# Attention and two MLPs on one core: SP's loads reordered, additions moved, x divided in place, and the query's low half later in VectorE's round

## The reference

```python
scores = scale * q @ k.T                    # causal
cum = cumsum(max(s, 0)); bias = min(-(cum[i] - cum[j]), 0)
attn = softmax(where(causal, -1e9, scores + bias))      # sum + 1e-9
x = (attn @ v) put back as (2304 tokens, 512)
h = x @ w_in; solu = h * softmax(h)                     # w_in 512 x 1024
x2 = ((solu - mean) / sqrt(var + 1e-6) * g_ln) @ w_out  # w_out 1024 x 512
y = max(x2 @ w1, x2 @ w2, x2 @ w3) @ w_out2             # w1..w3 512 x 768
```

## Time and profile before

| | us |
|---|---|
| three runs | 772.12, 773.01, 778.30 |
| median | 773.01 |
| profiled execution | 773.02 |
| its span (first to last instruction) | 771.2 |
| TensorE busy | 722.3 (94%) |
| VectorE, ScalarE, POOL busy | 394.9, 327.0, 251.4 |

### The profile page before, as it was taken

The page is one execution under the profiler, slowest core; times in us unless marked ns, Lnnn a source line. Parts: engine busy times, 40 slices in busy tenths (PEclk is TensorE's granted clock), DMA queues, the critical chain, the costliest instruction groups (busy, mean ns, idle before and its releaser), DMA issues.

```text
span 771.2 us, 12703 instructions
## 1 busy us (share of the span) xinstructions
PE 722.3 (94%) x4248; PEld 664.4 (86%) x4248; DVE 394.9 (51%) x702; ACT 327.0 (42%) x795; POOL 251.4 (33%) x248
## 2 busy tenths in 40 slices
PE   2799999999878899999999999999999999999997
PEld 2788888888767688989898989999989999899995
DVE  8898988888853675636354364612203213132120
ACT  1798888898853443424233242412112112121111
POOL 6766779888872842606040200000000000000000
PEclk9999999999998999999999999999999999999999
DMA  6598887878765312306100031000010000100101
GB/s 142 114 215 195 198 184 181 186 185 190 160 146 113 84 35 48 82 1 170 36 0 0 0 106 59 1 14 28 1 42 1 13 29 1 38 2 0 41 0 41
DMA packets 58227, 59.42 MB, mean 77 GB/s; under 512 B 23572, under 2 KB 45204, under 8 KB 58164
## 3 DMA queue, kind: packets, MB, share of 16 engines
q1 hardware_dynamic: 58196, 59.02, 32.0%
HBM read 44.15 MB, written 10.10 MB: 70 GB/s over the span
## 4 chain that ended last, share of the span: by engine, by line
PE 71%; DVE 8%; issue 6%; POOL 5%; DMA 4%; ACT 3%; SPq 2%; DVEq 0%; POOLq 0%; ACTq 0%
PE ps L652 10%; PE ps L653 10%; PE ps L651 10%; PE ps L584 4%; PE ps L586 4%; PE ps L585 4%; DMA qk_raw<-in_qk_dram 4%; PE ps L572 3%; PE ps L574 3%; PE ps L573 3%; PE ps L664 3%; PE ps L665 3%; PE ps L666 3%; PE ps L481 3%; DVE lnT_lo L1170 1%
## 5 line engine op out<-in xcount | busy, mean ns | idle before, releaser
L653 PE MATMUL ps<-x_lo,w_hi 128*128 (+1 forms) x432 | 144.4, 334 | 0.0
L651 PE MATMUL ps<-x_hi,w_hi 128*128 128x384 f32 x432 | 144.4, 334 | 0.0
L652 PE MATMUL ps<-x_hi,w_lo 128*128 128x384 f32 x432 | 144.4, 334 | 0.0
L481 PE MATMUL ps<-ident,probs 128*128 128x128 f32 x480 | 78.2, 289 | 21.9 <-DVE pt_lo L1069 15.6
L844 ACT ACTIVATE probs<-ps,nmax 128x576 f32<-128x576 f32 (+4 forms) x160 | 83.0, 539 | 17.7 <-DVE nmax L1062 17.5
L1069 DVE TENSOR_TENSOR pt_lo<-ps,pt_hi 128x512 fp32r<-128x512 f32 (+1 forms) x128 | 78.3, 652 | 11.6 <-ACT pt_hi L854 8.3
L481 PEld LDWEIGHTS ps<-ident,probs 128*128 128x128 f32 x480 | 52.4, 144 | 33.9 <-DVE pt_lo L1069 21.7
L651 PEld LDWEIGHTS ps<-x_hi,w_hi 128*128 128x128 f32 x432 | 81.1, 188 | 0.2
L652 PEld LDWEIGHTS ps<-x_hi,w_lo 128*128 128x128 f32 x432 | 81.1, 188 | 0.2
L653 PEld LDWEIGHTS ps<-x_lo,w_hi 128*128 128x128 f32 x432 | 81.1, 188 | 0.0
L854 ACT ACTIVATE pt_hi<-ps 128x512 fp32r<-128x512 f32 (+1 forms) x128 | 69.9, 572 | 26.4 <-PE ps L481 22.6
(11 more groups left out here) (101 smaller groups left out, 1436.3 us busy)
## 6 DMA issues: line engine op xcount, KB each, us to landing
qk_raw<-in_qk_dram SPq DMA_DIRECT2D x64, 288.0 KB, 4.4
xT<-halves SPq DMA_DIRECT2D x32, 144.0 KB, 2.5
xb_dram<-halves SPq DMA_DIRECT2D x32, 144.0 KB, 2.4
xb<-xb_dram SPq DMA_DIRECT2D x24, 192.0 KB, 3.9
rinvB<-rsum_dram SPq DMA_DIRECT2D x24, 192.0 KB, 4.1
stage<-in_moe_w_dram SPq DMA_DIRECT2D x18, 256.0 KB, 4.3
out_dram<-stage SPq DMA_DIRECT2D x18, 256.0 KB, 2.0
v_raw<-in_v_dram SPq DMA_DIRECT2D x32, 128.0 KB, 4.1
```

The source lines that it names most:

```text
L481: mm = pe.transpose(ps[:, GBANK[g], P * n:P * (n + 1)], probs[1 - par][:, o:o + P], ident[:, :])
L651: pe.matmul(dst, w_hi[f][:, i, c, :], x2_hi[par][:, c, :], start=(c == 0), stop=False)
L652: pe.matmul(dst, w_lo[f][:, i, c, :], x2_hi[par][:, c, :], start=False, stop=False)
L653: mm = pe.matmul(dst, w_hi[f][:, i, c, :], x2_lo[:, c, bass.ds(g * GT, GT)], start=False, stop=(c == KC - 1))
```

## The change

SP: aux(t-1) is loaded behind qk(t) and v(t-2), so SP no longer waits in `reload(t)` for the scores of head t-2. The list of the last heads is in another order. There are two `rinvB`, and `xg` is gone: `divide` writes back into `xT`, and no longer waits for `x_low`. POOL does round 30 before `join(0)`, and `divide(0)` before round 31. VectorE's `q_low(t+1)` stands behind `pt_low` 0 and 1.

```diff
@@ SP
+            def reload_aux(t, par):
+                sp.wait_ge(scores_done, 3 * (t - 1))
+                load_aux(t, par)
+
             def reload(t, par, known=None):
...
                 load_qk(t, par)
                 if known is None or known >= 4:
                     reload_v(t - 2, par)
-                if known == 2:
+                if known == 3:
                     sp.wait_ge(aux_stored, 16)
-                sp.wait_ge(scores_done, 3 * (t - 1))
-                load_aux(t, par)
+                if known is None or known >= 3:
+                    reload_aux(t - 1, 1 - par)
                 if known is None or known >= 5:
                     store_x(t - 5, 1 - par)
...
             reload(HEADS - 4, 0)
             load_xb(0)
             reload(HEADS - 3, 1)
             reload(HEADS - 2, 0)
+            reload(HEADS - 1, 1)
             sp.wait_ge(rinv_done, 1)
             store_rinv(slice(0, LAST))
-            reload(HEADS - 1, 1)
+            reload_aux(HEADS - 1, 1)
+            reload_v(HEADS - 2, 0)
+            store_x(HEADS - 5, 1)
             sp.wait_ge(rinv_stored, 16 * NCH)
             load_rinv(0)
-            load_xb(1)
-            reload_v(HEADS - 2, 0)
-            store_x(HEADS - 5, 1)
             reload_v(HEADS - 1, 1)
             store_x(HEADS - 4, 0)
+            load_rinv(1)
+            load_xb(1)
             store_x(HEADS - 3, 1)
+            store_x(HEADS - 2, 0)
             load_xb(2)
             sp.wait_ge(xg_ready, 1)
-            load_rinv(1)
-            store_x(HEADS - 2, 0)
+            load_rinv(2)
             store_x(HEADS - 1, 1)
             sp.wait_ge(rinv_done, 2)
             store_rinv(slice(LAST, HEADS))
             sp.wait_ge(rinv_stored, 16 * 2 * NCH)
-            for g in range(2, NG):
-                sp.wait_ge(xg_ready, g)
+            for g in range(3, NG):
+                load_xb(g)
+                sp.wait_ge(xg_ready, g - 1)
                 load_rinv(g)
-                if g + 1 < NG:
-                    load_xb(g + 1)
@@ POOL
-            def divide(g, known):
+            def divide(g, par):
                 cols = xT[:, :, bass.ds(g * GT, GT)]
-                pool.wait_ge(rinvB_loaded, 64 * (g + 1))
-                if known != 0:
-                    pool.wait_ge(x_lo_ready, 3 * g)
+                pool.wait_ge(rinvB_loaded[par], (g - par) * 32 + 64)
                 pool.wait_ge(x_added, g + 1)
-                pool.tensor_tensor(xg[:, :, :], cols, rinvB[:, :, :], ALU.mult).then_inc(xg_ready, 1)
+                pool.tensor_tensor(cols, cols, rinvB[par][:, :, :], ALU.mult).then_inc(xg_ready, 1)
...
+            slot(HEADS - 2, 0, HEADS - 2)
             join(0)
-            slot(HEADS - 2, 0, HEADS - 2)
+            divide(0, 0)
             slot(HEADS - 1, 1, HEADS - 1)
             join(1)
-            divide(0, 0)
             slot(HEADS, 0, HEADS)
-            divide(1, None)
+            divide(1, 1)
             join(2)
@@ VectorE
             def slot(t, par, known):
-                if live(known, -1):
-                    q_low(t + 1, 1 - par)
                 if live(known, 0):
                     row_max(t, par, 4)
                     row_max(t, par, 0)
                     row_max(t, par, 3)
                 if live(known, 1):
                     pt_low(0, t, par, known)
                     pt_low(1, t, par, known)
+                if live(known, -1):
+                    q_low(t + 1, 1 - par)
```

More of the change, by code:

```diff
@@ L111, in attention_and_mlp @@
         ab_.__enter__()
-        rinvB = sb(ab_, "rinvB", [P, KC, GT])
-        xg = sb(ab_, "xg", [P, KC, GT])
+        rinvB = [sb(ab_, f"rinvB{i}", [P, KC, GT]) for i in range(2)]
         xb = sb(ab_, "xb", [P, KC, GT])
@@ L220, in attention_and_mlp @@
         wout_lo_ready = sem("wout_lo_ready")
-        rinvB_loaded = sem("rinvB_loaded")
+        rinvB_loaded = [sem(f"rinvB_loaded{i}") for i in range(2)]
         xg_ready = sem("xg_ready")
@@ L393, in load_rinv @@
                         src = rsum_dram[HB * b_:HB * (b_ + 1), s0:s0 + GT // 2].rearrange("(j r) t -> r j t", r=2)[par:par + 1]
-                        dst = rinvB[D * par:D * (par + 1), :, part * GT // 2:(part + 1) * GT // 2]
-                        sp.dma_start(dst, src.broadcast_to([D, KC, GT // 2])).then_inc(rinvB_loaded, 16)
+                        dst = rinvB[g % 2][D * par:D * (par + 1), :, part * GT // 2:(part + 1) * GT // 2]
+                        sp.dma_start(dst, src.broadcast_to([D, KC, GT // 2])).then_inc(rinvB_loaded[g % 2], 16)
             LAST = HEADS - HB
@@ L811, in group @@
                 if more and not first:
-                    divide(g + 1, None)
+                    divide(g + 1, 1 - base)
                 for i in range(3):
@@ L911, in x_high @@
                     act.wait_ge(h_done, 3 * g + i - 1)
-                act.activation(x_hi[ab][:, :, :], xg[:, :, P * i:P * (i + 1)], ACT.Copy).then_inc(x_hi_ready, 1)
+                act.activation(x_hi[ab][:, :, :], xT[:, :, bass.ds(g * GT + P * i, P)], ACT.Copy).then_inc(x_hi_ready, 1)
             def gate(g, i, ab, first):
@@ L1122, in x_low @@
                 dve.wait_ge(x_hi_ready, 3 * g + i + 1)
-                dve.tensor_tensor(x_lo[ab][:, :, :], xg[:, :, P * i:P * (i + 1)], f32(x_hi[ab][:, :, :]),
+                dve.tensor_tensor(x_lo[ab][:, :, :], xT[:, :, bass.ds(g * GT + P * i, P)], f32(x_hi[ab][:, :, :]),
                                   ALU.subtract).then_inc(x_lo_ready, 1)
```

## The result

The changed kernel takes 784.9 us as a median of four runs, against 772.9: a ratio of 1.0132 (95% interval 1.0088 to 1.0175). It is slower, where 769.5 and a range to 777 were forecast. The profiled execution took 785.33 us with a span of 783.5, 12.3 us above the span before.

A forecast was written before the change was run, and what follows sets the result against it. TensorE was taken as full in both MLPs, leaving attention rounds and the passage out of them to gain from. 773.0 + 2.2 - 1.0 + 1.4 - 5.5 - 0.6 = 769.5 us; range 762 to 777.

The forecast's parts named there:

- part 5: Division in place and two rinvB: POOL's divisions start earlier, but TensorE is already busy afterwards; 0 us (-1 to +1).
- part 1: Attention rounds 4 to 26, q_low behind two subtractions: rounds of 6.55 us instead of 6.45; +2.2 us (-0.3 to +8).
- part 4: Passage out of attention, rounds 29 to 32: earlier loads and POOL's new order remove waits; -5.5 us (-8 to -2).
- part 3: Rounds 27 and 28: bias rows of head 28 land late behind the xb(0) loads; +1.4 us (0 to +2.5).
- part 2: Rounds 1 to 3, where first loads are late: TensorE gets the next scores' input sooner; -1.0 us (-2 to 0).
- the clock: With TensorE idling less, its granted clock should fall for less time; -0.6 us (-1.5 to 0).
- rival A: Every attention round is held by late q_low or late aux, 6.8 us each; total 776 us; chance 0.17.
- the 6.44 us: Counted length of an attention round once scores_4 waits for the moved q_low; no early load can shorten it.
- turning point: Round length in rounds 4 to 26, 6.70 us, above which the change would make the kernel slower.
- A's two causes: In attention rounds, scores_4 waits for q_low, which finds POOL's instruction in its way, or for late aux.
- the collision that was "near even": Round 30: if join(0) starts first, q_low(31) waits up to 3 us, losing 2.8 us of the passage's gain.
- The limit of 1.2 us: Longest hold of q_low by POOL's 3.49 us additions, allowed from rows of short instructions; the lock rule gave 3.4 us.

The follow-up runs named there:

- experiment 1: Changed kernel, but POOL's divisions of groups 2 to 5 again wait until x_low has read the group before: 778.8 us, ratio 1.0052 to the kernel before.
- experiment 5: Kernel before the change, with q_low alone moved behind the two subtractions: 774.4 us, ratio 0.9981.
- experiment 3: Changed kernel, but q_low back at the front of VectorE's round in all rounds: 767.8 us, ratio 0.9921 to the kernel before.
- Experiment 8: Changed kernel, but the four xb(0) loads issued two heads later, behind the loads of head 31: 783.1 us, ratio 1.0104 to the kernel before.
- experiment 9: Changed kernel, but q_low at the front of VectorE's round and later divisions waiting for x_low: 762.5 us, ratio 0.9824 to the kernel before.
- experiment 4: Changed kernel, but aux rows loaded as before, behind their own q and k and the scores wait; q_low late: 775.7 us, ratio 1.0029 to the kernel before.
- experiment 2: Changed kernel, but in round 30 alone q_low(31) is first in VectorE's round again: 780.5 us, ratio 1.0089 to the kernel before.

## Why the prediction was wrong

The direction was wrong; the mechanisms were nearly all named, with too small sizes or too small a chance. Forecast and trace lie 15.8 us apart: 5.6 in part 5, 4.0 in part 1, 2.9 in part 4, 2.0 in part 3, and 1.3 in part 2 and the clock.

**The step that failed is part 5.** "They now start ahead of a group's first normalization, while VectorE works from PSUM" holds from group 3 on. Group 2's division falls in the one place where VectorE has eight instructions with two SBUF operands, `wout_low`. Priced at 0 (-1 to +1), it cost 5.6 us from the first hidden matmul on, the clock with it; experiment 1 took 4.5 of them away. The pause (3.44 against 0.19 us) and the slower `second` block (10.9 against 8.6) add up to the 5.6. In the kernel before, the wait for x_low held this division back until `wout_low` was over. The prediction read it as a wait that "nothing is there to win" from, and did not ask what it kept apart, though the lock was on its own page.

**Part 1 was mis-sized, as rival A.** The step that was too small is the additions to the 6.44 us. The prediction took a third of the way up "since neither deficit need come in each round", 6.55, and the rounds were 6.72 in this trace and 6.63 to 6.83 in the four of the same work, around A's turning point of 6.70. What lengthens them is q_low, at 0.22 us a round; the late aux held one round, for 1.1 us. 23 x 0.22 + 1.1 = 6.2 us is nearly the whole excess over 23 x 6.44. So of A's two causes the first one acts, and the late aux acts mainly by when it lets POOL start. A's counter-argument, that POOL tends to start just after q_low, was true in four of 21 rounds; in eight it started 0.04 to 0.18 us before. With aux back the round was 6.53: for that kernel the 6.55 would have been right.

The floor came out, partly by luck: 6.44 counted, and the shortest round is 6.43 in the changed kernel and in experiment 1 and 6.42 in experiment 5, against 6.20 in the kernel before and in experiment 3. But the hop from q_low to the scores, put at 0.05 us without a row, is 0.43 to 0.49 in every round. Two things made up for it: q_low starts 3.3 us into its round, not 3.4, and from the scores to the next turn it is 1.95 us where the calm round had 2.27. That "everything behind it in the loop moves with it" was therefore not so: some 0.3 us came out of the stretch ahead of the next turn, where the calm round still waits 0.16 us for ScalarE.

The same placing of q_low also weighs on parts 3 and 4: by experiment 3 it costs 17 us in all, where part 1, its gain on late loads included, charged 2.2.

**Part 2** gained 0.35 of 1.0 us in this execution; starts scatter by more than that, so nothing is shown.

**Part 3** named the right cause and undersized it: +3.4 against +1.4. Experiment 8 brings round 27 from 9.06 to 6.82, so the loads behind xb cost 2.2 rather than 1.6 us in this trace (the growth of aux's landing, 0.5 to 1 us in the forecast, was not measured by itself). Round 28 was counted as 8.15 and took 9.71: the larger miss, and not taken apart. It takes 7.5 us in experiments 3 and 9, with q_low early, and 8.3 in experiment 4, so it, too, hangs on late q_low and late aux together.

**Part 4.** The order on POOL did what was counted: ScalarE no longer waits 3.22 us for the division, and rounds 29 to 32 got shorter. But the collision that was "near even" came: experiment 2 puts 4.5 us on round 30. With it, the forecast's own worse case was -4.8, and -2.6 was measured. The clock term of -0.6 did not come either: the granted clock in 190 to 240 us is 0.90 in both kernels. The lock rule of the Trainium skill ("SBUF — State Buffer", "SBUF: two separate sides"), held for the whole instruction, is what this case's rows show: 3.85 us beside an addition of 3.42. The limit of 1.2 us, taken from short instructions, is refuted.

What stays open: the interaction of 7.3 us between the two parts is shown by four kernels, and its size in other executions is not (one trace each). That POOL's q_a falls just ahead of q_low because SP waits for q_low was argued from durations and waits; no run shifts the one against the other. And what makes round 28 last 9.7 us.

## What to carry to other kernels

A stall that moves from one consumer to another isn't removed: before moving a step back behind others, find every reader of its result and its slack in the reader's own order; here moving TensorE's reader by 1.5 us did what moving the writer could not. When a wait is removed, look at what it kept apart, above all between two engines that exclude each other, and place the freed instruction by hand. And a load that waits for the same instruction that competes with its consumer can settle into a fixed phase, as the waits and starts here suggest: check whether that phase is the bad one.

## What was not expected of the hardware

A VectorE instruction of 0.76 us with two SBUF operands took 3.85 us beside one POOL addition of 3.42, and a chain of three of them 6.04 beside a normalization's tail and a division of 3.86. A pause of 3.4 us of TensorE in the middle of dense work was followed by a stretch at the lower clock in which a block of 8.6 us took 10.9: 2.3 us more for a pause of 3.4. That is not fixed: of the six traces with a pause of 3.3 to 3.5 us, five show 10.6 to 10.9 us for this block, and that of experiment 3 shows 8.6. There the granted clock fell as well (0.66 in 262 to 267 us), but was back at 1.00 in 267 to 272 us; the block starts at 267.62.
